# Two 64-row products at the end of each of the last 24 units of an mLSTM + two-layer MoE kernel on one core

## The reference, cut to what matters

```python
x = attn(q, k, v, i_gate, f_gate, o_gate)       # (1536 tokens, 320 features)
# layer 1
gate = 1 / (1 + exp(-(x @ w_gate)))             # w_gate, w_val: 320 x 1536
x = (gate * (x @ w_val)) @ w_out                # w_out: 1536 x 320
# layer 2
y = ((x @ w_a) * (x @ w_b)) @ w_out2            # 1536 x 320
```

## Time and profile before

| | |
|---|---|
| median of three runs | 464.91 us |
| profiled execution | 464.53 us, of which 462.8 us are the traced span |
| TensorE matmul busy | 456.6 us (99%), 2527 instructions |
| TensorE weight load busy | 403.3 us (87%) |
| VectorE busy | 206.6 us (45%) |
| ScalarE busy | 197.3 us (43%) |
| GpSimd busy | 88.4 us (19%) |
| mean granted TensorE clock | 1.00 |

### The profile page before, as it was taken

One profiled execution on the slowest core, in us unless ns is written; L12 is line 12 of the kernel. 1 busy time (PEld: TensorE's weight loads), 2 busy tenths in 40 slices (PEclk: granted clock), 3 DMA queues, 4 the chain that ended last, 5 costly groups with the idle time before them and its releaser, 6 DMA issues.

```text
span 462.8 us, 6645 instructions
## 1 busy us (share of the span) xinstructions
PE 456.6 (99%) x2527; PEld 403.3 (87%) x2527; DVE 206.6 (45%) x365; ACT 197.3 (43%) x362; POOL 88.4 (19%) x99
## 2 busy tenths in 40 slices
PE   8999999999999999999999999999999999999996
PEld 5888889898989889888889889988988998898896
DVE  8877886776465654343142253222323222322322
ACT  5965848658293745234253352213222221312222
POOL 4582322412403020002464260000000000000000
PEclk9999999999999999999999999999999999999999
DMA  5979495452533460001222300000100000100001
GB/s 155 263 245 274 155 291 186 147 158 84 152 102 105 132 219 1 1 1 48 97 97 87 107 1 0 1 1 0 36 22 1 1 1 0 58 0 1 0 1 57
DMA packets 22005, 38.06 MB, mean 82 GB/s; under 512 B 2910, under 2 KB 16225, under 8 KB 21973
## 3 DMA queue, kind: packets, MB, share of 16 engines
q1 hardware_dynamic: 21605, 36.58, 26.0%
q10 hardware_dynamic: 208, 0.71, 0.5%
q0 software_dynamic: 160, 0.35, 0.3%
HBM read 35.55 MB, written 2.04 MB: 81 GB/s over the span
## 4 chain that ended last, share of the span: by engine, by line
PE 93%; DVE 2%; ACT 2%; DMA 1%; issue 1%; POOL 0%; ACTq 0%; DVEq 0%; POOLq 0%
PE bank L580 56%; PE bank L597 27%; PE bank L502 4%; PE bank L493 1%; PE bank L468 1%; ACT pt L687 1%; PE bank L516 1%; PE bank L558 1%; PE bank L477 1%; PE bank L528 1%; DMA f_row<-f_in 1%; DVE w_lo L943 0%; DMA arow<-a_lo 0%; PE bank L440 0%; DVE q_stack L949 0%
## 5 line engine op out<-in xcount | busy, mean ns | idle before, releaser
L751 ACT CAST h_hi<-h_ff 128x512 fp32r<-128x512 f32 x72 | 44.6, 619 | 176.4 <-PE bank L597 95.2
L580 PE MATMUL bank<-xt,w_hi 128*128 128x512 f32 x360 | 118.1, 393 | 0.2 <-DVE w_lo L943 0.2
L968 DVE TENSOR_TENSOR h_lo<-h_ff,h_hi 128x512 fp32r<-128x512 f32 x72 | 52.0, 722 | 122.4 <-ACT h_hi L751 122.4
L962 DVE TENSOR_TENSOR h_ff<-bank,s_ff 128x512 f32<-128x512 f32 x72 | 49.7, 691 | 109.9 <-PE bank L580 104.0
L580 PE MATMUL bank<-xt,w_lo 128*128 128x512 f32 x216 | 84.3, 390 | 0.0
L580 PEld LDWEIGHTS bank<-xt,w_hi 128*128 128x128 f32 x360 | 66.2, 188 | 13.4 <-DVE t_st L930 0.4
L744 ACT ACTIVATE s_ff<-bank 128x512 f32<-128x512 f32 x72 | 43.0, 598 | 74.2 <-PE bank L580 73.2
L580 PE MATMUL bank<-xt,w_hi_mid 128*128 128x512 f32 x180 | 58.8, 391 | 0.0
L580 PE MATMUL bank<-xt,w_hi_end 128*128 128x512 f32 x180 | 58.8, 391 | 0.0
L580 PEld LDWEIGHTS bank<-xt,w_lo 128*128 128x128 f32 x216 | 40.5, 188 | 8.7
L597 PE MATMUL bank<-w_hi,h_hi 128*128 128x320 f32 x144 | 45.0, 312 | 0.0
(11 more groups left out here) (128 smaller groups left out, 683.9 us busy)
## 6 DMA issues: line engine op xcount, KB each, us to landing
w_raw<-w_in SPq DMA_DIRECT2D x24, 544.0 KB, 4.3
vk<-vk_in SPq DMA_DIRECT2D x12, 344.0 KB, 4.0
levels<-a_scratch SPq DMA_DIRECT2D x7, 512.0 KB
k_both<-kq_in SPq DMA_DIRECT2D x21, 120.0 KB
q_blk<-kq_in SPq DMA_DIRECT2D x21, 120.0 KB
y<-rows_t SPq DMA_DIRECT2D x12, 160.0 KB, 1.9
q<-kq_in SPq DMA_DIRECT2D x10, 180.0 KB
osig_b<-o_in SPq DMA_DIRECT2D x8, 160.0 KB, 2.7
```

The costliest lines, as they stand in the source:

```text
L580: mm = pe.matmul(up_bank(u, gv)[:, :], w_part(low, f, (gv * 3 + kt) * P, P), xt[:, xb * TOK + g * TG:xb * TOK + (g + 1) * TG], start=(j == ...
L751: act.copy(h_hi[u % 2][:, :], h_ff[u % 2][:, :]).then_inc(act_h, 1)
L962: dve.tensor_tensor(h_ff[u % 2][:, :], up_bank(u, 1)[:, :], s_ff[u % 2][:, :], ALU.mult).then_inc(dve_h, 1)
L968: dve.tensor_tensor(h_lo[u % 2][:, :], h_ff[u % 2][:, :], h_hi[u % 2][:, :].bitcast(F32), ALU.subtract).then_inc(dve_hlo, 1)
```

## The change

- From unit 48 on, a unit's up is `up_whole` for gate, `up_whole` for value (seven matmuls each, as before but without `(1, 2, 4)`), and then `up_halves`: two matmuls with 64 rows each. The gate's takes the low weights of rows 0 to 63 and the high inputs in rows 0 to 63. The value's takes the copy of the low weights in rows 64 to 127 and the high inputs from rows 64 to 127 of a new tile `x_twin`. Only these two signal `pe_g` and `pe_v`.
- `x_twin` lies over tiles that layer 2 doesn't need. ScalarE fills it with eight extra copies (64 partitions x 128), two in each of units 25, 26, 37, 38, ahead of `split_high`.
- From unit 48 on, odd units write their ups to the banks `XY`, even ones to `GB`, `VB`. So an up waits for the gate and the product of two units before, not one.
- From unit 47 on, the ups run two by two: up 48, up 49, down 47, 48, up 50, up 51, down 49, 50, to up 71, down 69, 70, 71.

```diff
--- before.py
+++ after.py
@@ -44,6 +44,7 @@
 UNITS = 2 * NG * NF
 ALONE = 4
 TRIPLE = 28
+PAIRED = 48
 RING = 3
 STACKED = 5
 LOW = -1.0e30
@@ -98,6 +99,8 @@
         def sem(name):
             return ctx.enter_context(nc.semaphore(name))
 
+        twins = []
+
         def chunk_set(stack, s):
 
             def ab(name, shape, dt=F32):
@@ -106,6 +109,10 @@
             rows = ExitStack()
             row_tile = rows.enter_context(nc.sbuf_tensor(f"arow{s}", [P, HEADS * P], F32R))
             rows.close()
+            if s == 0:
+                twin = ExitStack()
+                twins.append(twin.enter_context(nc.sbuf_tensor("x_twin", [P, (NG - 1) * TG], F32R)))
+                twin.close()
             return (ab("levels", [P, HEADS * P]), row_tile, ab("q_blk", [TRI, HEADS * P]), ab("k3_", [TRI, 3 * P]),
                     ab("q3_", [TRI, 3 * P]), ab("i_rep", [TRI, 3 * P]), ab("vk_", [P, VALL + 3 * TRI]),
                     ab("pt", [P, HEADS * P]), ab("x_raw", [P, DM]), ab("x_n", [P, 3 * P]),
@@ -138,6 +145,7 @@
         levels, arow, q_blk, k3, q3, i_rep, vk, pt, x_raw, x_n, den, rec = zip(set0, set1)
         w_hi, w_lo = sb("w_hi", [P, 6 * WC], F32R), sb("w_lo", [P, 6 * WC], F32R)
         xt = sb("xt", [P, 5 * TOK], F32R)
+        x_twin = twins[0]
         w_raw = [sb(f"w_raw{i}", [P, WC]) for i in range(RING)]
         ident = sb("ident", [P, P])
         osig_b = [sb("osig_b", [P, DM])] * 2
@@ -257,7 +265,7 @@
 
         def up_bank(u, gv):
 
-            return XY[gv] if u == UNITS - 1 else (GB, VB)[gv]
+            return XY[gv] if u >= PAIRED and u % 2 else (GB, VB)[gv]
 
         def next_turns(u):
 
@@ -560,6 +568,8 @@
 
             PASSES = ((0, 0, 0), (0, 0, 1), (1, 0, 0), (0, 1, 2), (0, 1, 3), (1, 1, 2), (0, 2, 4), (1, 2, 4))
 
+            WHOLE = tuple(x for x in PASSES if x != (1, 2, 4))
+
             def up(u, gv):
 
                 m, g, f = u // (NG * NF), u // NF % NG, u % NF
@@ -581,6 +591,32 @@
                                    xt[:, xb * TOK + g * TG:xb * TOK + (g + 1) * TG],
                                    start=(j == 0), stop=(j == len(PASSES) - 1))
                 mm.then_inc((pe_g, pe_v)[gv], 1)
+
+            def up_whole(u, gv):
+
+                m, g, f = u // (NG * NF), u // NF % NG, u % NF
+                if gv == 0 and f == 0:
+                    pe.wait_ge(dve_tr, BLK * (g + 1))
+                if gv == 0 and g == 0:
+                    pe.wait_ge(*split_done(NF * m + f))
+                if gv == 0 and u == PAIRED + 1:
+                    pe.wait_ge(dve_tr, NCH)
+                pe.wait_ge((act_s, dve_h)[gv], u if u == PAIRED else u - 1)
+                for j, (low, kt, xb) in enumerate(WHOLE):
+                    mm = pe.matmul(up_bank(u, gv)[:, :], w_part(low, f, (gv * 3 + kt) * P, P),
+                                   xt[:, xb * TOK + g * TG:xb * TOK + (g + 1) * TG],
+                                   start=(j == 0), stop=False)
+
+            def up_halves(u):
+
+                g, f = u // NF % NG, u % NF
+                for gv in range(2):
+                    part = slice(gv * KREM, (gv + 1) * KREM)
+                    side = (xt[part, 4 * TOK + g * TG:4 * TOK + (g + 1) * TG],
+                            x_twin[part, (g - 1) * TG:g * TG])[gv]
+                    mm = pe.matmul(up_bank(u, gv)[:, :], w_part(1, f, (gv * 3 + 2) * P, P)[part, :], side,
+                                   start=False, stop=True)
+                    mm.then_inc((pe_g, pe_v)[gv], 1)
 
             def down(u):
 
@@ -647,8 +683,13 @@
                 if k == 1 and n > ALONE:
                     scores(n, 0)
                     scores(n, 1)
-                up(u, 0)
-                up(u, 1)
+                if u < PAIRED:
+                    up(u, 0)
+                    up(u, 1)
+                else:
+                    up_whole(u, 0)
+                    up_whole(u, 1)
+                    up_halves(u)
                 if k == 2:
                     turn(n)
                     if n >= NCH - BLK:
@@ -660,6 +701,9 @@
                         down(u - 1)
                 elif u == UNITS - 1:
                     for v in range(u - 2, u + 1):
+                        down(v)
+                elif u >= PAIRED - 1:
+                    for v in range(u - 2, u) if u % 2 else ():
                         down(v)
                 elif (u - TRIPLE) % 3 == 2:
                     for v in range(u - 3, u):
@@ -838,7 +882,11 @@
                         split_high(act, turn_of_rows(0, tb), tb * P).then_inc(act_tr, 1)
                 for g, tb in next_turns(u):
                     act.wait_ge(pe_tr, BLK * g + tb + 1)
-                    split_high(act, turn_of_rows(g, tb), (BLK * g + tb) * P).then_inc(act_tr, 1)
+                    act.wait_ge(act_e, 2 * NCH)
+                    tp = turn_of_rows(g, tb)
+                    act.copy(x_twin[KREM:P, (BLK * (g - 1) + tb) * P:(BLK * (g - 1) + tb + 1) * P],
+                             tp[KREM:P, 2 * P:3 * P])
+                    split_high(act, tp, (BLK * g + tb) * P).then_inc(act_tr, 1)
                 for f in W_AT.get(u, ()):
                     w_high(f)
                 if 26 <= u < 26 + NF:
```

## The result

The changed kernel takes 468.07 us (median of 17 runs) against 464.23 us of the kernel before (17 runs): ratio 1.0075, 95% interval 1.0052 to 1.0098. It is slower by 3.8 us. The prediction said 471.0 us (463.0 to 475.5), 6.5 us slower. (Medians here are over all runs; ratios leave out runs more than 1.5% above the fastest of their kernel, one of e1 at 2070.89 us among them.)

A forecast was written before the change was run, and what follows sets the result against it. TensorE's matmul distances were taken as the bound. Two whole matmuls replaced by two halves, with a drain each way and exposed loads, add 0.27 us a unit, 24 times 6.5 us; from 464.53 that gives 471.0 us (463.0 to 475.5).

The forecast's parts named there:

- TensorE is the bound, and only its distances matter: Units 48 to 71: other engines wait for TensorE; only the distance between its matmuls counts, 0.227 us per up matmul.
- The drain at each change of rows: Around the halves TensorE empties its pipeline each way; first new load 0.32 us after the last old matmul's start.
- The first load exposed, 0.10 us: After each change of rows, the first weight load is not hidden and delays its matmul by 0.10 us.
- The second half 0.11 us behind the first: At each unit's end, the value's weights load and its half matmul starts 0.11 us after the gate's.
- its named lower bound: The unit sum with nothing exposed for the second half's load: 0.16 us more a unit, 3.8 us in all.
- both loads at once: Rival for the halves: drain present, second half starts with the first; 0.16 us a unit, 468.4 us, chance 0.15.
- the case held likeliest: Drain each way, second half 0.11 us late: 0.27 us more a unit, 6.5 us, 471.0 us, chance 0.40.
- up in the chain at 3.9 us: Sign in the profile after: up in units 48 to 71, 16 instructions, takes 3.9 us instead of 3.64.
- The gain: Rival: halves join the stream without emptying it and run at once; 5.5 us off, 459.1 us, chance 0.18.
- Late signals and banks: Signals at a unit's end cost nothing, as XY removes the wait; without it 1.3 us in each unit.
- Borders, end, twin copies: Adjoining downs 47/48 and 59/60, the tail after the last up, and ScalarE's extra copies cost nothing.

The follow-up runs named there:

- e1: Changed kernel with the two products at each unit's end on all 128 rows again, all else kept: 463.88 us, 0.9995 of the kernel before.
- e5: Changed kernel with halves and both bank pairs, but ups and downs by threes as in the kernel before: 468.09 us, 1.0088 of the kernel before.
- e4: Changed kernel with even units' halves last and odd units' first, so four stand together, one change there and back per two units: 463.82 us.
- e7: Changed kernel with each half directly behind its own seven whole matmuls, so 48 changes of rows there and back instead of 24: 483.88 us.
- e2: Changed kernel with both halves on rows 0 to 63, so they can't run at once; number of row changes kept: 474.03 us.
- e3: Changed kernel with the two products at the end left out in units 48 to 71, output incomplete: 453.73 us, 0.9780 of the kernel before.
- e6: Changed kernel without its second bank pair: even and odd units write the same two banks, unit 71 alone the others: 476.74 us.

## Why the prediction was right or wrong

**TensorE is the bound, and only its distances matter: right.** e1 and e5 show that nothing else of the change has a time of its own that could be seen: e1 is at 0.9995 of before (0.9976 to 1.0014), e5 within 0.02 us of the change.

**The drain at each change of rows: right, and shown.** It was read from four switches to and from 16 rows; for 64 rows the first load comes at 0.32 us as predicted, and the load behind the halves 0.07 us before their end. The times of e4 and e7 follow the number of changes: 12, 24 and 48 of them at 0.40 to 0.44 us each. That TensorE empties its pipeline there is read from where the loads start; the price is measured, and the 0.41 us there and back include the weight loads that the change exposes.

**The first load exposed, 0.10 us: right.** Half matmuls 0.50 us by their record against 0.39 for whole ones, and 0.11 us at the first matmul behind.

**The second half 0.11 us behind the first: wrong, and the step of the sum that failed.** The prediction gave it "the value's weights load 0.11 us later, and its matmul goes at 0.53 beside the first". Both loads start at 356.78 and both matmuls too; in all 24 units the two are 3 to 4 ns apart by the trace's times in ns. The 0.11 us holds for loads on the same rows (e2). The sum without it is 0.16 us a unit, 3.8 us, its named lower bound and the rival "both loads at once" at 468.4 us, with a chance of 0.15; measured were 468.07. The argument against that rival ("every pair of loads in the trace is 0.11 us apart") came from pairs on the same rows and said nothing about different ones. So the case held likeliest, 471.0 us at 0.40, did not come true.

**Size.** The chain gives 0.20 us a unit where loads at once gave 0.16. 0.02 of the difference stands in the steps (0.86 - 0.68 = 0.18: each exposed load took 0.11 us, where the sum had 0.10); the other 0.02 is spread over the first matmuls behind a change, and its reason is open. The sign "up in the chain at 3.9 us" came out as 3.63 us for an even unit (3.20 + 0.43) and 3.83 for an odd one (3.40 + 0.43), since the cost of the way back falls on what follows: on the odd unit's up, or on the 24 downs (3.72 for 3.52).

The whole time grew by less than the 4.7 us of the units: 0.7 us less is left behind the last copy and 0.6 us less was spent ahead of 218 us. All eight kernels that were built from the change, it included, have 2.8 to 2.9 us behind the start of that copy; only the kernel before has 3.5. The medians point the same way: e4's units take as long as those of before and e1's 0.02 us a pair longer, and both are 0.5 to 0.6 us under it. So the kernel before is probably some 0.6 us longer outside these units; the reason is open. The prediction has no term for it. That the sum with loads at once (3.8 us) meets the 3.8 us between the medians is therefore partly luck: it is 0.9 us short on the units, and the rest of the kernel made up for it.

**The gain: excluded.** e3 shows that some 5.4 us were there to be had (half of the 10.7 that leaving both products out gives), and e2 that the overlap was had. The 24 changes there and back, 24 x 0.41 = 9.8 us, cost more than that.

**Late signals and banks: right that they cost nothing, wrong in the price without cover.** It was put at 1.3 us in each unit; e6 shows 0.76 us, in odd units alone. An even unit follows downs, which hide it, and the value half never waits.

**Borders, end, twin copies: right.** Behind unit 49, where down 47 and down 48 adjoin, the 24 downs take 3.72 us as everywhere (the chain at 334.92), and so they do behind unit 61. The last 36 downs show no wait. e1 carries all three and has the time of before.

```profile
334.92 3.72 PE bank L633 x24
...
457.90 5.49 PE bank L633 x36
```

**The chances.** Slower by over 1% had 0.52 and within 1% 0.31; it came out at 0.75%, in the second. The range of 8 in 10 (463.0 to 475.5 us) holds the measured 468.07.

## What to carry to other kernels

Two half-height matmuls at once gave back one matmul's time here (e2, which runs them in turn, took 5.4 us more over 24 units, 0.23 each), but a change of rows there and back cost 0.41 us, 1.8 matmuls of 512 columns. So a single pair between two changes lost 0.20 us a unit, and two pairs side by side broke even (e4, 10.79 us a pair of units as before). That longer runs of halves would gain is an estimate from this price; more than two pairs side by side were not tried. Gather all small-row work between two changes before counting the gain. Where signals move to the end of a block, price the missing bank by who waits first and in which blocks, not by the whole chain: in e6 that was 0.76 us in odd units alone, where the prediction had 1.3 us in each.

## What the runs showed of the hardware

- A matmul call on fp32r tiles is one matmul record with one weight load: 48 calls of three units are 48 records in 10.90 us, 0.227 us each, and 120 such matmuls have 120 loads.
- Two weight loads on different 64-row parts start at the same time (356.78 and 356.78), two on the same rows 0.11 us apart (e2).
- Between two pairs of halves side by side the pipeline isn't emptied: e4's second pair of loads starts 0.11 us after the first (363.49 and 363.38), beneath its matmuls (363.38 to 363.87).
- The first load after a change stands 0.07 to 0.08 us before the recorded (modelled) end of the last matmul on the old rows, in both directions: for 16 rows at 8.09, 8.31, 20.90 and 21.50, for 64 rows at 356.78 and 357.21 in the change.
- A change of rows there and back costs 0.40 to 0.44 us beyond the matmuls' own time (the change, e2, e4, e7; 12, 24 and 48 changes).
